# A third buffer for q and k and a second one for v in two places that are free for a while

## What is computed

```python
scores = matmul(q_c, k_c.T) / sqrt(64); attn = softmax(scores); out = matmul(attn, v_c)
x = out.transpose(0, 2, 1, 3).reshape(4608, 512)
xn = x / sqrt(mean(x * x) + 1e-6) * rms_g                       # first network
x = (silu(xn @ w_gate) * (xn @ w_val)) @ w_out
h = x @ w_in2; out = (h * clip(h + 3, 0, 6) / 6) @ w_out2       # second network
```

## The kernel before

| pair | scores | probs. turned | attend | x turned |
|---|---|---|---|---|
| 8 | 7 | 9 | 14 | 20 |
| 9 | 12 | 15 | 21 | 24 |
| 10 | 18 | 23 | 26 | 31 |
| 11 | 24 | 28 | 33 | 37 |
| 12 | 32 | 37 | 39 | 44 |
| 13 | 40 | 43 | 46 | 50 |

## Time and profile before

### The profile page before, as it was taken

How to read it: one execution, slowest core, us unless ns; L and a number is a source line. 1 busy time by engine, 2 the same in 40 slices (tenths; PEclk the granted TensorE clock), 3 DMA queues, 4 the chain that set the end, 5 groups by cost and what they waited for, 6 DMA issues and landing times.

```text
span 1649.5 us, 29728 instructions
## 1 busy us (share of the span) xinstructions
PE 1605.6 (97%) x11335; PEld 1569.5 (95%) x11337; DVE 1047.5 (64%) x1441; ACT 858.5 (52%) x1341; POOL 786.9 (48%) x772
## 2 busy tenths in 40 slices
PE   7889999999999999999999999999999999999998
PEld 5678999899999999999999999999999999999998
DVE  4878877868754556655554776665666765455454
ACT  4666766655544444544444665555655644434432
POOL 2543543449786654434340376777676630231231
PEclk9999999999999999999999999999999999999999
DMA  9577777554566555989997856656658986776674
GB/s 177 133 170 184 176 201 173 143 159 155 167 229 208 195 205 184 366 311 310 311 316 275 304 210 238 210 183 246 227 189 274 372 275 204 220 230 210 212 227 119
DMA packets 335646, 366.88 MB, mean 222 GB/s; under 512 B 186256, under 2 KB 299152, under 8 KB 332304
## 3 DMA queue, kind: packets, MB, share of 16 engines
q1 hardware_dynamic: 321584, 334.69, 64.3%
q0 software_dynamic: 8800, 28.85, 5.1%
q10 hardware_dynamic: 5120, 1.44, 0.5%
HBM read 200.80 MB, written 164.10 MB: 221 GB/s over the span
## 4 chain that ended last, share of the span: by engine, by line
PE 85%; DVE 3%; issue 3%; ACT 2%; DMA 2%; POOL 2%; SPq 2%; ACTq 0%; DVEq 0%; POOLq 0%
PE bx L968 14%; PE by L968 14%; PE bx L970 13%; PE by L970 13%; PE bx L969 13%; PE by L969 13%; DMA hl_b<-h_scratch 1%; SPq L568 1%; PE att L937 1%; PE att L946 1%; PE att L895 1%; DMA hl_d<-u_scratch 1%; PE att L918 1%; DVE wr L1511 1%; DVE tx L1498 1%
## 5 line engine op out<-in xcount | busy, mean ns | idle before, releaser
L968 PE MATMUL by<-tx,wr 128*128 128x384 f32 x840 | 286.2, 341 | 2.7 <-ACT vb L1176 1.0
L968 PE MATMUL bx<-tx,wr 128*128 128x384 f32 x840 | 285.8, 340 | 2.7 <-ACT gb L1176 1.2
L970 PE MATMUL bx<-tx,wr 128*128 128x384 f32 x840 | 281.4, 335 | 0.0
L970 PE MATMUL by<-tx,wr 128*128 128x384 f32 x840 | 281.3, 335 | 0.0
L969 PE MATMUL by<-tx,wr 128*128 128x384 f32 x840 | 281.2, 335 | 0.0
L969 PE MATMUL bx<-tx,wr 128*128 128x384 f32 x840 | 281.2, 335 | 0.0
L1549 DVE TENSOR_TENSOR hl_d<-hl_d 128x1536 fp32r<-128x1536 f32 x84 | 146.2, 1774 | 94.0 <-ACT hl_d L1248 93.9
L1867 POOL DMA_DIRECT2D out_dram<-ot x128 | 70.2, 556 | 248.3 <-DVE ot L1572 245.8
L1549 DVE TENSOR_TENSOR hl_b<-hl_b 128x1152 fp32r<-128x1152 f32 x84 | 118.9, 1431 | 106.1 <-ACT hl_b L1248 105.3
L1248 ACT ACTIVATE hl_d<-hl_d 128x1536 fp32r<-128x1536 f32 x84 | 123.3, 1486 | 113.7 <-DMA hl_d<-u_scratch 113.4
L968 PEld LDWEIGHTS by<-tx,wr 128*128 128x128 f32 x840 | 158.0, 188 | 7.2 <-DVE ub L1523 1.9
(11 more groups left out here) (193 smaller groups left out, 3773.3 us busy)
## 6 DMA issues: line engine op xcount, KB each, us to landing
hl_d<-u_scratch SPq DMA_DIRECT2D x84, 768.0 KB, 4.4
hl_b<-h_scratch SPq DMA_DIRECT2D x84, 576.0 KB, 5.7
u_scratch<-ut SPq DMA_DIRECT2D x48, 576.0 KB, 3.7
h_scratch<-ht SPq DMA_DIRECT2D x36, 576.0 KB, 3.6
u_scratch<-ub SPq DMA_DIRECT2D x96, 192.0 KB, 2.8
u_scratch<-ub SPq DMA_DIRECT2D x48, 384.0 KB, 2.5
h_scratch<-vb SPq DMA_DIRECT2D x72, 192.0 KB, 3.5
h_scratch<-vb SPq DMA_DIRECT2D x36, 384.0 KB, 3.1
```

The source lines that it names most:

```text
L968: pe.matmul(dst, w_hi, m_hi, start=start, stop=False, skip_group_check=not opens)
L970: return pe.matmul(dst, w_lo, m_hi, start=False, stop=stop, skip_group_check=not opens)
```

## The change

`qk_b`, a third buffer of q and k, lies in the place in `wr` that unit 5 of the weights will take, and so does `v_b`, a second one of v. `qk_b` serves n2 = 5 alone, `v_b` pairs 7 and 9. `v_c` takes over from `v_b` for pairs 11, 13, ...; it lies where `w_sum_a` was, and is first loaded at slot 28, when the low part of unit 5 is done. So each v is loaded one pair ahead of before, in the slot in which the pair before it used to be loaded. The load of n2 = 6 (pairs 12 and 13) starts at slot 10, not 19, that of n2 = 7 at slot 27, not 26. Since unit 5 now has to wait for the buffers in its place, its high parts move from slots 20 and 24 to 23 and 25, its low parts from 24 and 26 to 25 and 27, and the first high part gets three waits.

```diff
+    qk_b = at("qk_b", [P, 2, 2 * D], F32, W0 + 71680)
     qk_c = at("qk_c", [P, 2, 2 * D], F32, U0 + 82944)
     v_a = at("v_a", [P, H, DH + 1], F32, U0 + 94208)
+    v_b = at("v_b", [P, H, DH + 1], F32, W0 + 79872)
+    v_c = at("v_c", [P, H, DH + 1], F32, U0 + 91136)
...
+    V_C, V_C_SLOT = 11, 28
...
     def qk_buf(n):
         n2 = n // 2
-        return 1 if n2 >= 7 and n2 % 2 == 1 else 0
+        return 2 if n2 == 5 else n2 % 2
...
-    QK_FIRST = {5: (5, 2), 6: (19, 2), 7: (26, 2), 8: (41, 2)}
+    QK_FIRST = {5: (5, 2), 6: (10, 2), 7: (27, 2), 8: (41, 2)}
...
+    def v_buf(n):
+        return 0 if n % 2 == 0 else 1 if n < V_C else 2
...
+    def v_slot(n):
+        return V_C_SLOT if n == V_C else at_slot_of(n - 2, AT) + 1
...
-    HI_AT = {2: ((0, 3), (0, 4)), 3: ((0, 9), (0, 10)), 4: ((1, 2), (1, 2)), 5: ((1, 6), (1, 10)),
+    HI_AT = {2: ((0, 3), (0, 4)), 3: ((0, 9), (0, 10)), 4: ((1, 2), (1, 2)), 5: ((1, 9), (1, 11)),
...
-    LO_AT = {2: ((0, 6), (0, 6)), 3: ((0, 9), (0, 12)), 4: ((1, 4), (1, 4)), 5: ((1, 10), (1, 12)),
+    LO_AT = {2: ((0, 6), (0, 6)), 3: ((0, 9), (0, 12)), 4: ((1, 4), (1, 4)), 5: ((1, 11), (1, 13)),
...
-                elif part == 0 and n2 >= 5:
-                    sp.wait_ge(q_transposed, n if n2 in (5, 6) else n - 2)
-                    sp.wait_ge(k_transposed, n if n2 in (5, 6) else n - 2)
+                elif part == 0 and n2 >= 6:
+                    sp.wait_ge(q_transposed, n - 2)
+                    sp.wait_ge(k_transposed, n - 2)
...
         def load_v(n):
             t, p = tp_of(n)
-            if n > NG:
-                sp.wait_ge(attn_done, n)
+            if n == V_C:
+                sp.wait_ge(w_lo, part_no(UA2 - 1, 1))
+            elif n > NG + 1:
+                sp.wait_ge(attn_done, n - 1)
...
         load_v(NG)
+        load_v(NG + 1)
         load_qk(4)
...
-                n = woven(m, slot, AT, 1)
-                if n is not None and n + 1 < NN:
-                    load_v(n + 1)
+                for n in range(NG + 2, NN):
+                    if v_slot(n) == 14 * m + slot:
+                        load_v(n)
...
+            if u == UA2 - 1 and part == 0:
+                act.wait_ge(q_transposed, 12)
+                act.wait_ge(k_transposed, 12)
+                act.wait_ge(attn_done, 10)
             act.activation(parts_to(u, part)[:, :, HI], blocks_of(u, part), ACT.Copy).then_inc(w_hi, 1)
...
+                if (m, slot) == (2, 0):
+                    pool.wait_ge(w_lo, part_no(UA2 - 1, 1))
+                    pool.memset(v_c[:, :, DH:DH + 1], 1.0).then_inc(v_ones, 1)
```

More of the change, by code:

```diff
@@ L196, in chunked_attention_then_two_ffns @@
     g_loaded = sem("g_loaded")
-    q_loaded = [sem("q_loaded_a"), sem("q_loaded_c")]
-    k_loaded = [sem("k_loaded_a"), sem("k_loaded_c")]
-    v_loaded = sem("v_loaded")
+    q_loaded = [sem("q_loaded_a"), sem("q_loaded_c"), sem("q_loaded_b")]
+    k_loaded = [sem("k_loaded_a"), sem("k_loaded_c"), sem("k_loaded_b")]
+    v_loaded = [sem("v_loaded_a"), sem("v_loaded_b"), sem("v_loaded_c")]
+    v_ones = sem("v_ones")
     q_loaded_first = [sem(f"q_loaded_first{n}") for n in range(NQ)]
@@ L320, in t_no @@
         return 4 * m + place + 1 if m < B0 else 4 * B0 + 8 * (m - C0) + 2 * place + st + 1
+    V_C, V_C_SLOT = 11, 28
     def qk_buf(n):
         n2 = n // 2
-        return 1 if n2 >= 7 and n2 % 2 == 1 else 0
+        return 2 if n2 == 5 else n2 % 2
     def qk_loads(n):
         n2 = n // 2
-        return (n2 - 5) // 2 if qk_buf(n) == 1 else n2 - 3 if n2 <= 6 else n2 // 2
+        return (n2 // 2 - 1, (n2 - 5) // 2, 1)[qk_buf(n)]
     def qk_of(n):
         which, full = qk_buf(n), 16 * (P // TB) * (CH // TB) * qk_loads(n)
-        return (qk_a, qk_c)[which], n % 2 * D, (q_loaded[which], full), (k_loaded[which], full)
-    QK_FIRST = {5: (5, 2), 6: (19, 2), 7: (26, 2), 8: (41, 2)}
+        return (qk_a, qk_c, qk_b)[which], n % 2 * D, (q_loaded[which], full), (k_loaded[which], full)
+    QK_FIRST = {5: (5, 2), 6: (10, 2), 7: (27, 2), 8: (41, 2)}
     def qk_slots(n2):
@@ L341, in qk_slots, with v_loads @@
         return [first + i // each if i < 14 else first + i - 14 if each == 1 else first + i // each for i in range(16)]
+    def v_buf(n):
+        return 0 if n % 2 == 0 else 1 if n < V_C else 2
+    def v_loads(n):
+        return (n - NG) // 2 + 1 if v_buf(n) < 2 else (n - V_C) // 2 + 1
+    def v_slot(n):
+        return V_C_SLOT if n == V_C else at_slot_of(n - 2, AT) + 1
     def v_of(n):
-        return v_first[n // 2][:, n % 2 * H:(n % 2 + 1) * H, :] if n < NG else v_a[:, :, :]
+        return v_first[n // 2][:, n % 2 * H:(n % 2 + 1) * H, :] if n < NG else (v_a, v_b, v_c)[v_buf(n)][:, :, :]
     def fill_no(f, o):
@@ L548, in load_qk @@
             t, p = tp_of(n)
-            buf, which = (qk_a, qk_c)[qk_buf(n)], qk_buf(n)
+            buf, which = (qk_a, qk_c, qk_b)[qk_buf(n)], qk_buf(n)
             for part in parts:
@@ L588, in load_v @@
             t, p = tp_of(n)
-            if n > NG:
-                sp.wait_ge(attn_done, n)
+            if n == V_C:
+                sp.wait_ge(w_lo, part_no(UA2 - 1, 1))
+            elif n > NG + 1:
+                sp.wait_ge(attn_done, n - 1)
+            vv = (v_a, v_b, v_c)[v_buf(n)]
             for e in range(2):
-                sp.dma_start(v_a[e * CH:(e + 1) * CH, :, 0:DH],
-                             v[2 * p:2 * p + 2].rearrange("c (j e) s d -> e s (c j) d", e=2)[e, t * CH:(t + 1) * CH]).then_inc(v_loaded, 16)
+                sp.dma_start(vv[e * CH:(e + 1) * CH, :, 0:DH],
+                             v[2 * p:2 * p + 2].rearrange("c (j e) s d -> e s (c j) d", e=2)[e, t * CH:(t + 1) * CH]).then_inc(v_loaded[v_buf(n)], 16)
         def store_x(s, a):
@@ L929, in attend @@
             else:
-                pe.wait_ge(v_loaded, 32 * (n - NG + 1))
+                pe.wait_ge(v_loaded[v_buf(n)], 32 * v_loads(n))
+                if n == V_C:
+                    pe.wait_ge(v_ones, 1)
             pe.wait_ge(probsT_copied, n + 1)
@@ L1875, in _ @@
             pool.memset(const, value).then_inc(consts_ready, 1)
-        for vv in (v_first[0], v_first[1], v_first[2], v_a):
+        for vv in (v_first[0], v_first[1], v_first[2], v_a, v_b):
             ones = pool.memset(vv[:, :, DH:DH + 1], 1.0)
```

## The result

| | before | after |
|---|---|---|
| median of 12 runs each, same chip | 1652.42 us (1647.89 to 1655.28) | 1644.95 us (1642.39 to 1650.85) |
| ratio | | 0.9965, 95% interval 0.9954 to 0.9975 |
| profiled execution (span) | 1651.29 us (1649.5) | 1644.85 us (1643.1) |

By the ratio the change wins 5.8 us (4.1 to 7.6); the two medians alone lie 7.5 us apart. The prediction said 3.6 and a range, 1644.3 to 1653.2, that holds 1644.95 near its lower end. On a second chip, with 12 runs of the changed kernel and 26 of before, the ratio was 0.9969 (0.9951 to 0.9988).

The account below looks back on a forecast made before the run. TensorE is busy for 97% of the span, so only idle time can be won. Terms 1.6 + 1.4, then 3.44 less the new wait of 2.4, less 0.4, give 3.6 us: 1649.1 us, range 1644.3 to 1653.2.

Parts of the forecast that it names:

- The queue up to unit 5: SyncE's loads: k of `qk_b` there by 82.4 us, removing VectorE's 1.66 us wait; unit 5's raw weights land at 88.7.
- transpose_x(9): Wait there shrinks through GpSimd's earlier sums and shorter `inverse_rms(9)`: 1.6 us won, bounds 0.6 and 2.1.
- hidden anyway: Rival: unit 5's raw weights land at 89.9 or later, gain only 1.5 us, 1651.2 us; chance 0.14.
- scores(12) and attend(12): TensorE's waits ahead of these, 1.42 us from VectorE's wait for k and 3.44 us for v(12), both go.
- first term: The gain at `transpose_x(9)`, taken as 1.6 us between 0.6 and 2.1.
- attend(11): v(11), behind unit 5's second low part, is issued at 104.3 us, not 108.67; hidden by 1.4 us, no wait.
- The new wait: Ahead of `transpose_probs(13)`, TensorE waits 2.4 us for ScalarE's exponentials, leaving 4.0 us won there.
- The extra v load: One more v load ahead of `qk_a`'s first loads near 37 us costs nothing; uncovered it would cost 1.3 us.
- The likeliest case: Whole kernel: the forecast itself, 2 to 5 us won, 1647.7 to 1650.7 us; chance 0.52.
- second rival: Raw weights of unit 5 land late and waits only get other names: 1.5 us won, 1651.2 us; chance 0.14.
- More is won: Rival: no delay by row sums and exponentials at `transpose_probs(13)`, gain 6.4 to 6.9 us, 1645.8 to 1646.3; chance 0.27.
- Slower: Rival: unit 5's second low part late, delaying v(11) and `attend(11)`; slower from 5 us of delay on; chance 0.07.

Follow-up runs that it names:

- late_n2_6: The changed kernel with the q and k loads of pairs 12 and 13 issued from slot 19, as before, not 10; ratio 0.9966 to the kernel before.
- qk_only: The changed kernel with only one v buffer, keeping the third q and k buffer and unit 5's later slots; ratio 0.9970 to the kernel before.
- v_only: The changed kernel with q and k buffers and early slots as before, keeping the extra v buffers and unit 5's later slots; ratio 0.9997 to the kernel before.
- front_only: The kernel before with v(7) alone in a buffer of its own, loaded at the start; ratio 1.0001 to the kernel before.
- re_after: The changed kernel unaltered, run again on another chip; ratio 0.9969 to the kernel before.
- shift_only: The kernel before with only unit 5's high and low parts moved to their later slots; ratio 1.0016 to the kernel before.
- rms_first: The kernel of best with `inverse_rms(12)` one slot earlier on GpSimd, ahead of the sum waiting for a store; ratio 0.9941 to the kernel before.
- re_before: The kernel before unaltered, profiled again on another chip; 80.24 us from the start of `transpose_probs(8)` to that of `transpose_x(14)`, against 78.68.
- late_lo: The changed kernel with unit 5's second low part two slots later; profile only, 77.68 us from `transpose_probs(8)` to `transpose_x(14)`, against 75.29.
- best: The changed kernel with third q and k load nine steps later, second operand's fill two slots later, unit 5's first high part one slot earlier; ratio 0.9959.

## Why the prediction was right, step by step

Both traces counted from the start of `transpose_probs(8)` give, for each place of the replay, what was won in all up to there:

| up to the start of | before | after | won | predicted |
|---|---|---|---|---|
| `transpose_x(9)` | 25.28 | 24.06 | 1.2 | 1.6 |
| `scores(12)` | 37.46 | 34.87 | 2.6 | 3.0 |
| `attend(12)` | 51.03 | 44.72 | 6.3 | 6.4 |
| `transpose_probs(13)` | 56.77 | 53.18 | 3.6 | 4.0 |
| `transpose_x(13)` | 68.22 | 64.82 | 3.4 | 3.6 |

*The queue up to unit 5: right in k, late in the raw weights.* The last k load of `qk_b` is issued by 76.9, and VectorE waits for none. The second of the raw weights was issued at 83.26, which is 12.1 us from the landmark, as replayed (85.0 less 72.95). But the sums could start only 16.70 us from it where 15.85 were replayed (88.8 less 72.95): the weights took 4.5 us to land, not 3.7 (from 83.26 to 87.8).

*transpose_x(9): one half right, the other mis-sized.* The term was 1.6 between 0.6 and 2.1, from a start 1.1 us earlier and an `inverse_rms` up to 1.0 shorter. The second came in full (1.54 to 0.55). The start moved by 0.24 (before, 89.89 less 72.95 is 16.94), for want of the raw weights; late_n2_6 gives them room and has the 15.66. The sum of 1.2 is what the table has. The condition that "hidden anyway" named for the raw weights (89.9 or later, 16.95 from the landmark) was missed by only 0.25 us; what it left out is that the short `inverse_rms` comes all the same. That 1.2 of 1.6 us came is in part luck: almost all of it is the half that was held to be the less certain one.

*scores(12) and attend(12): right.* The 0.4 of the first term is carried along to `scores(12)`. At `attend(12)` it is hidden: 3.7 us were won between the two, not 3.4, in part since before also had 0.16 us of a wait ahead of `attend(11)` that the replay left out. *attend(11): right.* v(11) went out at 102.79, 31.7 us from the landmark, 31.35 replayed, and nothing waits. The second low part ended at 101.85, 30.7 from it, where 103.1 replayed is 30.15. The sum behind that (102.73, 1 us later, 1.6 won) gives 102.1 and not the "102.5 at best" of the text; the value taken was the safer one, and still 0.6 too early.

*The new wait: right in place and cause, 1.68 us for 2.4.* TensorE comes to it 1.15 us later than replayed (122.62 is 51.50 from the landmark, 123.3 replayed is 50.35). A wait of 0.57 us for VectorE at 121.28 is part of that; at `attend(12)` it was only 0.1 late. The exponentials end 0.4 later than replayed.

*Whose waits they were.* The replay gave the 0.69 and 3.44 us to the earlier loads of v. qk_only shows that the third buffer of q and k frees the queue and with it v, so the v buffers are not needed for these waits. v_only shows that they take these two waits away as well, but that others take their place and no time is won. That attribution was wrong, the sum was not.

*The extra v load: "nothing" was right, as far as front_only can tell.* In the profiles before and after F differs by 1.06 us, but re_after has 19.06 again and shift_only, without the load, 18.02.

*The total: 3.6 predicted, 3.4 in S, 5.8 in the ratio.* In the profiled pair, 6.4 us of span are 0.8 ahead of F, 1.1 in F, 3.4 in S, 0.7 given back up to the first read of `hl_b`, and 1.8 behind it. The 0.8 and 1.1 are not the change's: re_after has 0.15 and none. Behind `hl_b`'s first read, where no instruction was moved, the profiles of this study take from 975.3 to 985.2 us, in no relation to S (977.2 and 977.8 before, 975.3 both times after, 981.6 in late_n2_6 and 982.5 in rms_first). The replay was made from an execution in which S was 1.6 us shorter than in re_before, and no fall of the clock is in its S. Against re_before, after and re_after are 4.95 and 4.6 us shorter in S, so that 3.6 and 3.4 agree within 0.2 us is in part luck.

What makes up the 2.2 us between 3.6 and 5.8 stays open; the interval begins at 4.1. A candidate that the prediction did not have is TensorE's clock. It fell behind the waits at `scores(12)` and `attend(12)` in three of the four profiles that have them as before has, and behind the one at `transpose_probs(13)` in three of the six that have it at 1.7 us; the fall cost 1.3 us in re_before (28.96 less 27.65) and 0.2 in re_after (22.30 less 22.11). The mean granted clock of the runs is 0.9946 for 35 of before and 0.9960 for 12 of late_n2_6 on one chip, 0.9942 for 26 of before and 0.9948 for 12 of after on another; as an estimate, 0.001 of 1650 us is 1.65 us. But v_only has 0.9953 beside that 0.9946 and gains nothing. No run here separates it.

The likeliest case (2 to 5 us won) ended short, and by the prediction's own bound of 5 us the result is just on the faster side, to which it gave 0.27. That 1644.95 lies inside the range is in part luck too: no case gave a time under 1645.8, and only the allowance of 1.5 us for the spread takes the range to 1644.3. The text says that the range goes from the second rival's far side; by its numbers it is the first one's.

*The rivals.* "More is won" gave 1645.8 to 1646.3, next to the measured median, but not by its mechanism: `transpose_probs(13)` does wait. It takes the further changes of rms_first to win 6 us in S. "Hidden anyway" did not come: the first term was 1.2, not 0. "Slower" was tried in late_lo, and another instruction than v(11) waits first.

## What to carry to other kernels

When several waits for DMA stand in one queue, look for the first load that was issued late; the ones behind it inherit its lateness. Here a buffer for them bought no time (v_only, 0.9997) and one for the first bought all that was to be had (qk_only, 0.9970). Replay a change by offsets from a common landmark and stop at the next chain that does not move: here 2.7 us of what `attend(12)` had won came back behind it, 1.68 of them as a wait for ScalarE. When a wait moves on from one engine to the next, follow it to the instruction that it ends at: in best it was one GpSimd instruction standing behind another that waited for a store. And before two single profiles are compared, look at TensorE's clock in short windows: a fall of 3.4 us can be as large as the difference.
